# Hashing in eight array tiles, a shorter way to the exponential's bias, and two pieces of vector work moved between blocks

## The reference

```
q_bits = (q @ proj > 0); k_bits = (k @ proj > 0)        # proj is 64 x 6
q_bucket = sum(q_bits * 2**arange(6)); k_bucket likewise
scores = where(q_bucket == k_bucket, scale * q @ k.T, -1e9)
attn = exp(scores - max(scores)); attn /= sum(attn) + 1e-9
out = attn @ v
```

## Time and profile before

| | |
|---|---|
| runs | 453.7, 452.68, 452.4 us; median 452.68 us |
| the profiled execution | 453.35 us, its span 451.6 us, mean granted TensorE clock 0.996 |
| busy: PE, PEld | 439.5 us (97%), 321.0 us (71%) |
| busy: DVE, ACT, POOL | 281.9 us (62%), 240.8 us (53%), 131.7 us (29%) |
| chain of waits, by engine | PE 92%, DVE 4%, ACT 2%, DMA 1%, issue 1% |

### The profile page before, as it was taken

The page is one execution under the profiler, slowest core; times in us unless marked ns, Lnnn a source line. Parts: engine busy times, 40 slices in busy tenths (PEclk is TensorE's granted clock), DMA queues, the critical chain, the costliest instruction groups (busy, mean ns, idle before and its releaser), DMA issues.

```text
span 451.6 us, 8054 instructions
## 1 busy us (share of the span) xinstructions
PE 439.5 (97%) x2887; PEld 321.0 (71%) x2887; DVE 281.9 (62%) x595; ACT 240.8 (53%) x485; POOL 131.7 (29%) x101
## 2 busy tenths in 40 slices
PE   7899999999999999999989999999999999999996
PEld 5776767767677676776756654366888888888885
DVE  2777776767667676676752611049997676557661
ACT  5688777787778787787873411047332312222211
POOL 3477555775557755577000000000000000000000
PEclk9899999999999999999999999999999999999999
DMA  5454543545535455357518389991000200020002
GB/s 176 163 173 161 184 153 132 164 157 184 160 127 166 157 181 171 119 170 245 178 39 304 159 324 399 408 390 65 1 1 1 93 1 0 2 93 1 1 0 93
DMA packets 27512, 64.29 MB, mean 142 GB/s; under 512 B 2912, under 2 KB 7008, under 8 KB 26976
## 3 DMA queue, kind: packets, MB, share of 16 engines
q1 hardware_dynamic: 27200, 63.38, 40.4%
q10 hardware_dynamic: 288, 0.59, 0.4%
HBM read 57.87 MB, written 3.15 MB: 135 GB/s over the span
## 4 chain that ended last, share of the span: by engine, by line
PE 92%; DVE 4%; ACT 2%; DMA 1%; issue 1%; SPq 0%; ACTq 0%
PE ps L573 17%; PE ps L593 15%; PE ps L583 13%; PE ps L831 9%; PE ps L833 9%; PE ps L832 9%; PE ps L754 3%; PE ps L735 3%; PE ps L563 3%; PE ps L558 2%; PE ps L810 2%; PE ps L662 1%; ACT arena L852 1%; DVE low_raw L982 1%; DMA arena<-in_qk 1%; PE ps L602 1%
## 5 line engine op out<-in xcount | busy, mean ns | idle before, releaser
L982 DVE TENSOR_REDUCE low_raw<-ps 128x1 f32<-128x768 f32 x96 | 91.6, 954 | 57.9 <-PE ps L573 56.0
L852 ACT ACTIVATE arena<-ps,exp_bias,exp_scale 128x768 f32<-128x768 f32 x96 | 95.2, 991 | 18.3 <-DVE exp_bias L987 17.4
L573 PE MATMUL ps<-stack_b,stack_a 96*128 96x384 f32 (+1 forms) x384 | 92.9, 364 | 2.9 <-ACT arena L852 2.9
L846 ACT COPY arena<-ps 128x384 f32<-128x384 f32 x160 | 69.9, 478 | 32.4 <-PE ps L583 32.3
L573 PEld LDWEIGHTS ps<-stack_b,stack_a 96*128 96x128 f32 (+1 forms) x384 | 63.3, 191 | 31.2 <-ACT arena L852 18.2
L583 PE MATMUL ps<-const,arena 128*128 128x128 f32 x576 | 79.6, 274 | 1.3 <-ACT arena L846 1.3
L831 PE MATMUL ps<-w_high,g_high 128*128 128x512 f32 x192 | 75.0, 391 | 1.2 <-DVE g_low L1137 1.2
L833 PE MATMUL ps<-w_high,g_low 128*128 128x512 f32 x192 | 74.7, 389 | 0.0
L832 PE MATMUL ps<-w_low,g_high 128*128 128x512 f32 x192 | 74.7, 389 | 0.0
L583 PEld LDWEIGHTS ps<-const,arena 128*128 128x128 f32 x576 | 69.2, 141 | 5.3 <-ACT arena L852 1.5
L960 ACT ACTIVATE arena<-ps 128x512 f32<-128x512 f32 x48 | 28.3, 599 | 79.6 <-PE ps L810 79.6
(11 more groups left out here) (110 smaller groups left out, 410.4 us busy)
## 6 DMA issues: line engine op xcount, KB each, us to landing
ring_lo<-in_moe_w SPq DMA_DIRECT2D x6, 2048.0 KB, 12.2
ring_lo<-in_moe_w SPq DMA_DIRECT2D x12, 1024.0 KB, 5.4
arena<-in_qk SPq DMA_DIRECT2D x31, 384.0 KB, 3.4
arena<-in_moe_w SPq DMA_DIRECT2D x3, 2048.0 KB, 8.1
out<-ring_lo SPq DMA_DIRECT2D x12, 256.0 KB, 2.1
arena<-in_v SPq DMA_DIRECT2D x15, 192.0 KB, 2.4
x_sb<-in_moe_w SPq DMA_DIRECT2D x1, 2048.0 KB, 8.9
ring_lo<-in_moe_w_in SPq DMA_DIRECT2D x1, 2048.0 KB, 22.3
```

Source lines behind the costliest of these rows:

```text
L573: last = nc.tensor.matmul(s_ps[p % 2][:, c, :], a[r][0:used, rows], b[r][0:used, cols], start=(a is stack_a1), stop=(a is stack_a2))
L846: nc.scalar.copy(probs_t[:, place(r, p), b * HALF:(b + 1) * HALF, :], ring[b].rearrange("p (a s) -> p a s", a=HALF)).then_inc(t_taken[b], 1)
L852: nc.scalar.activation(probs[:, p % 2, :].rearrange("p (c s) -> p c s", c=2), s_ps[p % 2], ACT.Exp, bias=exp_bias[:, r, p:p + 1], scale=ex ...
L982: nc.vector.tensor_reduce(low, s_ps[p % 2], axis=AX.XY, op=ALU.min).then_inc(min_found, 1)
```

## The change

The edits:

- `hashes` makes eight matmuls of 64 rows, 32 output partitions and 192 columns in place of four of 128 rows and 384 columns. Rows 0 to 63 make the first half of the columns and rows 64 to 127 the second; `proj_w` holds proj in both halves. The results go to the first 192 columns of banks 6 and 7, so the hashes now share bank 6 with `o_ps`.
- For that, TensorE waits before the hashes for `x_scaled`, and before the first half of `times_v` for `hash_taken`. The waits of the hashes are placed before the last transpose of the fifth block.
- `mins` forms the bias straight from the minimum, (low < EMPTY) * low, and then the scale, without a wait between them.
- `LATE` becomes (0, 2, 4): in the fifth block DVE copies the second half.
- DVE's `take_hashes` goes from the fifth to the sixth block.
- POOL does `low_k` before `scale_bits`.

```
--- before.py
+++ after.py
@@ -186,7 +186,7 @@
         s_ps = [ps[:, 2 * w:2 * w + 2, 0:HC] for w in range(2)]
         ring = [ps[:, 4 + b, 0:HC] for b in range(2)]
         o_ps = ps[:, 6, 0:HC]
-        hash_ps = ps[:, 7, 0:HC]
+        hash_ps = ps[:, 6:8, 0:HC // 2]
 
 
         ones_set = sem("ones_set")
@@ -208,7 +208,6 @@
         t_taken = [sem(f"t_taken{b}") for b in range(2)]
         scores_ready = sem("scores_ready")
         min_found = sem("min_found")
-        scale_found = sem("scale_found")
         min_ready = sem("min_ready")
         probs_ready = sem("probs_ready")
         o_ready = sem("o_ready")
@@ -286,7 +285,7 @@
 
             return not isinstance(m, int) or 0 <= m + ahead < HEADS
 
-        LATE = (0, 2)
+        LATE = (0, 2, 4)
 
         def place(r, p):
 
@@ -536,9 +535,11 @@
                         .then_inc(q_high, 1)
                     high_k(r, both)
                     low_q(m + 2, r, both)
+                    pool.wait_ge(q_low, m + 3)
+                    low_k(m + 2, r, both)
+                    pool.wait_ge(k_low, m + 3)
                     scale_bits(m + 2)
                     pool.wait_ge(bits_scaled, m + 2)
-                    low_k(m + 2, r, both)
                     nc.gpsimd.tensor_tensor(stack_b2[r][lower, :], both[lower, 1, :], over(k_scale, lower), ALU.mult)\
                         .then_inc(k_again, 1)
 
@@ -560,8 +561,11 @@
             def hashes(src):
 
                 for j in range(NQ):
-                    last = nc.tensor.matmul(hash_ps[j * QUAD:(j + 1) * QUAD, :], proj_w,
-                                            src[:, j % 2, (j // 2) * HC:(j // 2 + 1) * HC], start=True, stop=True)
+                    for y in range(2):
+                        rows = slice(y * D, (y + 1) * D)
+                        first = (j // 2) * HC + y * (HC // 2)
+                        last = nc.tensor.matmul(hash_ps[j * QUAD:(j + 1) * QUAD, y, :], proj_w[rows, :],
+                                                src[rows, j % 2, first:first + HC // 2], start=True, stop=True)
                 last.then_inc(hash_ready, 1)
 
             def scores(m, r, p):
@@ -574,12 +578,14 @@
                                                 start=(a is stack_a1), stop=(a is stack_a2))
                 last.then_inc(scores_ready, 1)
 
-            def transpose_probs(m, p):
+            def transpose_probs(m, p, meanwhile=lambda: None):
                 for b in range(2):
                     if not isinstance(m, int) or m * TILES + p > 0:
                         pe.wait_ge(t_taken[b], m * TILES + p)
                     for j in range(HALF):
                         kt = b * HALF + j
+                        if kt == TILES - 1:
+                            meanwhile()
                         last = nc.tensor.transpose(ring[b][:, j * P:(j + 1) * P], probs[:, p % 2, kt * P:(kt + 1) * P],
                                                    ident[:, :])
                     last.then_inc(t_ready[b], 1)
@@ -630,19 +636,27 @@
                     pe.wait_ge(probs_ready, m * TILES + p + 1)
                     if p + 2 < TILES or within(m, 1):
                         scores(*target(m, r, k, p))
-                    transpose_probs(m, p)
+                    hashing = p == TILES - 2 and within(m, 2)
+
+                    def hashes_can_run():
+                        if hashing:
+                            pe.wait_ge(qk_in[r], (k + 2) * 2 * DMA)
+                            pe.wait_ge(hash_taken, m + 2)
+                            if within(m, -1):
+                                pe.wait_ge(x_scaled, m)
+
+                    transpose_probs(m, p, hashes_can_run)
                     if p == 0 and within(m, -1):
                         pe.wait_ge(v_in[1 - r], (k + r) * DMA)
+                        pe.wait_ge(hash_taken, min(m + 2, HEADS) if isinstance(m, int) else m + 2)
                         times_v(m - 1, 1 - r, 0)
                     if p == 2 and within(m, -1):
                         times_v(m - 1, 1 - r, 1)
                     if p == HALF and within(m, -1):
                         transpose_o(m - 1)
-                    if p == TILES - 2 and within(m, 2):
-                        pe.wait_ge(qk_in[r], (k + 2) * 2 * DMA)
-                        pe.wait_ge(hash_taken, m + 2)
+                    if hashing:
                         hashes(both)
-                    if p == TILES - 1 and within(m, -1):
+                    if p == TILES - 1 and within(m, -1) and not within(m, 2):
                         pe.wait_ge(x_scaled, m)
 
             heads(pe, body)
@@ -981,15 +995,13 @@
                 low = low_raw[:, r, p:p + 1]
                 nc.vector.tensor_reduce(low, s_ps[p % 2], axis=AX.XY, op=ALU.min).then_inc(min_found, 1)
                 dve.wait_ge(min_found, g + 1)
+                nc.vector.tensor_scalar(exp_bias[:, r, p:p + 1], low, EMPTY, low, ALU.is_lt, ALU.mult)
                 nc.vector.tensor_scalar(exp_scale[:, r, p:p + 1], low, EMPTY, -1.0, ALU.is_lt, ALU.mult)\
-                    .then_inc(scale_found, 1)
-                dve.wait_ge(scale_found, g + 1)
-                nc.vector.tensor_scalar(exp_bias[:, r, p:p + 1], low, exp_scale[:, r, p:p + 1], -1.0, ALU.mult, ALU.mult)\
                     .then_inc(min_ready, 1)
 
             def take_hashes():
 
-                nc.vector.tensor_scalar(bits[:, :], hash_ps, 0.0, bit_less, ALU.is_gt, ALU.subtract)\
+                nc.vector.tensor_scalar(bits[:, :].rearrange("p (y n) -> p y n", y=2), hash_ps, 0.0, bit_less, ALU.is_gt, ALU.subtract)\
                     .then_inc(hash_taken, 1)
 
             def norm(m, r):
@@ -1033,7 +1045,7 @@
                         norm(m - 1, 1 - r)
                     if p == HALF and within(m, -1):
                         scale_o(m - 1, 1 - r, k + r - 1)
-                    if p == TILES - 2 and within(m, 2):
+                    if p == TILES - 1 and within(m, 2):
                         dve.wait_ge(hash_ready, m + 3)
                         dve.wait_ge(bits_in[1 - r], (k + 1) * NQ * DMA)
                         take_hashes()
@@ -1177,6 +1189,7 @@
     at = P + slots
     for c in (0, bits):
         consts[0:d, at + c:at + c + bits] = proj
+        consts[d:2 * d, at + c:at + c + bits] = proj
     at += quad
     scale = 1.0 / float(np.sqrt(d))
     consts[0:d, at], consts[d:, at] = 1.0, -scale

```

15 lines of the change are left out of this document (7 added, 8 removed).

## The result

The changed kernel takes **460.32 us** (median of 4 runs, 459.57 to 460.91) against 452.54 us for the kernel before (4 runs, 452.04 to 453.7): ratio 1.0161, 95% interval 1.0146 to 1.0176. It is 7.8 us slower, where 4.5 us faster was forecast. The profiled execution's span is 457.8 us.

A forecast was written before the change was run, and what follows sets the result against it. TensorE's sequence and a DVE-ACT chain tied at 3.72 us per head. Gains of 14 x 0.24 + 0.2 + 0.12 + 0.9 = 4.6, rounded to 4.5 us, from a 452.68 us median gave 448.2 us, range 446.2 to 451.2.

The forecast's parts named there:

- POOL and SP: scale_bits behind low_k moves the bits' DMAs and the load of q and k by about 0.7 us; both hidden.
- The step on the hash: On TensorE, eight half-width tiles cut each hash from 0.78 to 0.48 us, saving 0.30, with the doubled loads hidden.
- rival B: TensorE's hash gets no shorter: row halves take turns or loads lose their cover; about 452.0 us; chance 0.11.
- The tie: From tile 0's to tile 2's scores, TensorE's sequence and the DVE-ACT chain both take 3.72 us; after, 3.42 and 3.48.
- the bias: On DVE, bias straight from the minimum brings min_ready 0.12 us earlier per tile, counted twice in the chain: 0.24.
- The half tile on DVE: In the fifth block ACT loses a 0.43 us copy, else it holds the chain at 3.72; DVE's 0.55 costs nothing.
- The bits in the sixth block: DVE's 0.62 us moves behind tile 1's minimum; TensorE waits for it before times_v; margin 0.2 us, no cost.
- rival C: DVE's bits come late and times_v starts 0.45 us late: 2.4 us slower, 455.1 us; chance 0.06.
- The start: Before the regular heads: 0.6 us from the shorter first hash plus earlier first exponentials, together 0.9 us (0.3 to 1.6).
- The sum of the gain: Over the kernel, 14 x 0.24 + 0.2 + 0.12 + 0.9 = 4.6 us, rounded to 4.5.
- A: The forecast itself, 448.2 us, own range 446.4 to 450.6; chance 0.80.
- D: On TensorE, eight loads side by side fail and run in single file: 13 us slower, 466; chance 0.03.

The follow-up runs named there:

- experiment 5: Kernel after, POOL's new order kept, with SP's load of q and k put ahead of the bits' DMAs: 453.89 us, ratio 1.0032.
- experiment 2: Kernel after with only POOL's order undone (scale_bits before low_k again): 448.35 us, ratio 0.9895 to the kernel before.
- Experiment 6: Kernel of experiment 2 with the hashes as four matmuls of 128 rows and 384 columns again: 452.24 us, ratio 0.9997 to the kernel before.
- experiment 7: Kernel of experiment 2 with scale, wait and bias one after the other as before: 453.16 us, ratio 1.0011 to the kernel before.
- experiment 8: Kernel of experiment 2 with LATE back to (0, 2), so ACT copies both halves: 448.06 us, ratio 0.9902 to the kernel before.
- experiment 4: Kernel after with stack_b2 before scale_bits on POOL and the load of q and k before the bits on SP: 448.5 us, ratio 0.9901.
- `tiles_bias`: Kernel before plus only eight-tile hashes and bias straight from the minimum, with the waits on the last transpose: 448.26 us, ratio 0.9903.
- experiment 10: Kernel after with the piece of the experts' weights issued from ACT's queue at the fifth block's end: 457.54 us, ratio 1.0105.

## Why the prediction was wrong

**The step that failed is "POOL and SP".** It had the mechanism in hand (scale_bits behind low_k, four DMAs, the load behind them) and called it hidden. Three things in it were wrong.

*Sizes.* The load was said to move by 0.7 us. Against POOL's start it moved by 1.10, from 116.17 - 107.03 = 9.14 us in the kernel before to 10.24 in the kernel after. In experiment 5, where the load stands first in the queue, it goes out after 9.25: so 0.1 us of that is POOL's own and 1.0 the wait behind the bits' DMAs. It was said to land 0.5 + 3.4 us after its issue; to the point where POOL starts it takes 4.3 to 4.9, once 5.9.

*The deadline.* The sum set the landing, 120.8, against the hash at 123.26. The load's first customer is POOL, which started at 107.03 and 121.17 in the kernel before. With the true sizes the load is there for POOL at 116.17 + 1.10 + 4.3 = 121.6 at best, and with 4.9 at 122.2, and POOL starts late. In the kernel before 9.14 + 4.3 to 4.9 makes 13.4 to 14.0 us, just within a head.

*The shape.* Above all, a late start of POOL is not absorbed. POOL's start decides the next load, and that the next start. A ring longer than the head drifts against TensorE by its excess on every turn. The trace shows it drift: POOL's starts at 34.70, 49.59 and 64.75 us stand 1.67, 0.62 and 0.04 us ahead of TensorE's hashes at 36.37, 50.21 and 64.79. By the third the margin is used up, and from there TensorE runs at the ring's pace. POOL's starts from 34.70 to 214.30 are 12 turns in 179.6 us, 14.97 each. The eleven from TensorE's hash at 50.21 to that at 214.53 take 164.3 us, where experiment 2 takes 152.2 (51.17 to 203.38): that is 12.1 us more. The kernel after was 1.0 us ahead at the first of these hashes, so 11.1 are left, the difference between the spans of the two profiled executions (457.8 and 446.7).

**The step on the hash held**, to a hundredth: 0.48 forecast, 0.49 measured, loads hidden. Experiment 6 shows that without it a head is back at 14.06 to 14.14 us. The Trainium skill (TensorE: Matmul & The Clock Gate, Part 3) says that weight loads overlap matmuls in flight only when their row groups differ. The trace does not agree: four tiles of the same rows stand side by side in each half, yet the sixteen loads of one hash take 0.18 us together, and the hash holds TensorE for 0.49 us, not for the 0.78 of rival B.

**The tie and the bias held.** Chain 3.72 us with the old bias (experiment 7), 3.42 to 3.5 with the new; each part without the other gains nothing. The head of 13.79 us came out as 13.8 to 13.9 wherever the ring did not bind, and the time of 448.2 as 447.8 to 448.5. The saving per head was 0.23 us: by the starts of its hashes a head of the kernel before takes 14.07 us, not 14.03, and one of experiment 2 13.84.

**The half tile on DVE** was read wrongly, as needed to free ACT: it is worth nothing (experiment 8). **The bits in the sixth block** cost nothing that the runs can tell (experiments 2 and 4): rival C, to which I gave the slower side, did not occur, and TensorE did not wait for DVE's bits as it foresaw.

**The start.** The 0.6 us taken for the first hash is met: it holds TensorE for 0.83 us in the kernel after (5.76 to 6.59), 1.44 before (5.98 to 7.42). That the clock was at its lower level there is not shown, since the profile gives it as 1.00 from 0 to 16 us; only the long records speak for it. The third hash starts at 22.21 us in the kernel after, 24.78 before, more than the 0.9 us forecast, but how much of that is the edits' is open: from 17 to 19 us the granted clock was 0.50 in the profile of the kernel before (TensorE had stood still from 12.9 to 14.8) and 1.00 in that of the kernel after, and `tiles_bias`, which has both parts that carry the gain, had 0.50 from 16 to 18 us and its third hash at 24.51.

**The sum of the gain** is met partly by luck. In the profile of experiment 2 the third hash starts 1.64 us earlier than before (23.14 against 24.78), where 0.9 was forecast for the start, and the 13 heads from there to the last hash give 2.65 us, where 13 x 0.24 would be 3.1. (A's own range is also 0.2 us too wide at both ends: 452.68 less 2.3 and less 6.1 is 450.4 and 446.6.)

**None of the rivals was this one.** B, C and D all stood on TensorE and DVE. For those two engines I had asked what is late next when a stall goes; for the queue that the change moved I had not.

**The low clock.** Behind the five transposes of 166.70 the sixth waited 2.21 us for the load. TensorE then stood still from about 167.4 to 169.6, and from there to about 176 us the granted clock was 0.50. From the hash at 170.02 to times_v at 176.23 TensorE took 6.21 us, where it had taken 113.01 - 109.55 = 3.46 four heads earlier, so 2.75 more. None of it is left at the end of attention. The hash at 170.02 stood 0.22 us behind POOL's start, the next at 186.61 stood 1.99 behind, then 1.15 (200.49 against 199.34), and the last at 214.53 again 0.23, since POOL's turns went on at 14.7 to 15.0 us. The runs agree: the one with this clock loss (mean 0.993) took 459.57 us, one with a mean of 0.999 took 460.12. The turn that led to it took 16.2 us, with the load landing for POOL only 5.9 us after its issue; why is open.

## What to carry to other kernels

When a change moves a step, follow its semaphores and its queue until they come back to it. If they do, it is a ring: add up one turn and compare it with the period of the loop, not one landing with one deadline, since an excess that looks small against a margin is paid on every turn once the margin has drifted away. A queue shared by two transfers has two deadlines; ask for both before swapping them. And where two chains tie, an edit that shortens only one measures as nothing: try them together before dropping either.

## What the runs showed of the hardware that I had not expected

- Eight tiles of 64 rows and 32 columns run side by side. Sixteen records of 192 columns hold TensorE for 0.49 us, end included, where eight of 384 took 0.78.
- ACT starts an exponential 0.12 us before the record of the copy ahead of it ends (107.14 against 107.26), as DVE's minimum starts 0.09 early in the earlier trace rows (108.85 against 108.94). A record's end is not the earliest start of the next.
- The load of q and k landed for POOL 4.3 to 4.9 us after its issue in the kernel after, over some heads by turns (4.35, 4.89, 4.33), and once after 5.9. With the weights moved away it was still 4.2 to 5.2 (experiment 10). The cause is open.
